# Attention and two feed-forward layers on one core: whole-tile query and key loads, sink values loaded head by head, and moved splits

## The reference

```python
# attention: q, k, v (2, 8, 768, 64); n_sink 4, window 128
scores = scale * np.matmul(q, k.transpose(0, 1, 3, 2))
keep = (pos[None, :] < n_sink) | ((rel >= 0) & (rel < window))
a = softmax(np.where(keep, scores, -1e9)); attn = np.matmul(a, v)
x = attn.transpose(0, 2, 1, 3).reshape(1536, 512)
# first layer: w_in (512, 1024), w_out (1024, 512)
h = x @ w_in
solu = h * softmax(h)
x = ((solu - mu) / np.sqrt(var + 1e-6) * g_ln) @ w_out
# second layer: w2_in (512, 2048), w2_out (2048, 512)
r = np.maximum(x @ w2_in, 0.0)
return (r * r) @ w2_out
```

## Time and profile before

| | us |
|---|---|
| median of 3 runs | 504.93 |
| lowest, highest | 503.52, 505.35 |
| the profiled execution's own time | 503.79 |
| its span | 502.1 |

### The profile page before, as it was taken

The page is one execution under the profiler, slowest core; times in us unless marked ns, Lnnn a source line. Parts: engine busy times, 40 slices in busy tenths (PEclk is TensorE's granted clock), DMA queues, the critical chain, the costliest instruction groups (busy, mean ns, idle before and its releaser), DMA issues.

```text
span 502.1 us, 7334 instructions
## 1 busy us (share of the span) xinstructions
PE 484.4 (96%) x2644; PEld 393.3 (78%) x2644; DVE 287.0 (57%) x513; ACT 201.1 (40%) x532; POOL 95.5 (19%) x138
## 2 busy tenths in 40 slices
PE   8989989999999999999789999999999999999997
PEld 6667667888778888877678888888888888888885
DVE  4999898888898887865693433332222232232222
ACT  3667546545665655433343322421211232221121
POOL 2555051120022202357970000000000000000000
PEclk9999999999999999999999999999999999999999
DMA  8921343452222211038100000020000002000002
GB/s 247 289 66 44 113 146 80 121 162 62 55 61 75 60 40 35 14 84 290 22 4 0 1 0 1 0 84 0 0 0 0 0 0 85 0 1 0 0 1 84
DMA packets 39717, 29.21 MB, mean 58 GB/s; under 512 B 29256, under 2 KB 29256, under 8 KB 39176
## 3 DMA queue, kind: packets, MB, share of 16 engines
q1 hardware_dynamic: 39384, 28.56, 19.6%
q10 hardware_dynamic: 304, 0.27, 0.2%
HBM read 22.52 MB, written 3.15 MB: 51 GB/s over the span
## 4 chain that ended last, share of the span: by engine, by line
PE 76%; DVE 14%; SPq 5%; ACT 2%; issue 2%; POOL 1%; DMA 0%; DVEq 0%; POOLq 0%; ACTq 0%
PE score_ps L1407 24%; PE h_ps L1419 12%; PE h_ps L1214 9%; PE w_ps L1252 7%; PE wt_ps L1419 6%; PE w_ps L1419 6%; SPq L342 4%; PE o_ps L1184 2%; PE score_ps L1156 2%; PE wt_ps L1164 1%; DVE prob L905 1%; PE wt_ps L1156 1%; DVE bstat L862 1%; SPq L399 1%; DVE u L855 1%
## 5 line engine op out<-in xcount | busy, mean ns | idle before, releaser
L1407 PE MATMUL score_ps<-x2T_hi,w2in_hi 128*128 (+1 forms) x192 | 74.8, 389 | 0.0
L1407 PE MATMUL score_ps<-x2T_hi,w2in_lo 128*128 (+1 forms) x192 | 74.7, 389 | 0.0
L1407 PE MATMUL score_ps<-x2T_lo,w2in_hi 128*128 (+1 forms) x192 | 74.7, 389 | 0.0
L1089 DVE TENSOR_TENSOR sq<-relu 128x512 f32<-128x512 f32 x24 | 18.6, 775 | 83.2 <-ACT relu L775 83.2
L1089 DVE TENSOR_TENSOR e<-e 128x512 f32<-128x512 f32 x24 | 18.5, 770 | 79.6 <-ACT e L775 79.6
L775 ACT ACTIVATE relu<-score_ps 128x512 f32<-128x512 f32 x24 | 14.4, 598 | 100.0 <-PE score_ps L1407 100.0
L775 ACT ACTIVATE e<-score_ps 128x512 f32<-128x512 f32 x24 | 14.4, 599 | 90.4 <-PE score_ps L1407 90.4
L1407 PEld LDWEIGHTS score_ps<-x2T_hi,w2in_lo 128*128 128x128 f32 x192 | 36.1, 188 | 7.5
L1407 PEld LDWEIGHTS score_ps<-x2T_hi,w2in_hi 128*128 128x128 f32 x192 | 36.0, 188 | 7.5
L1407 PEld LDWEIGHTS score_ps<-x2T_lo,w2in_hi 128*128 128x128 f32 x192 | 36.0, 188 | 7.3
L600 ACT ACTIVATE prob<-sm,nbias 128x132 f32<-128x132 f32 (+1 forms) x96 | 37.8, 396 | 0.5
(11 more groups left out here) (177 smaller groups left out, 1094.8 us busy)
## 6 DMA issues: line engine op xcount, KB each, us to landing
w2in<-w_in SPq DMA_DIRECT2D x4, 1024.0 KB, 5.1
w2out<-w_out SPq DMA_DIRECT2D x8, 512.0 KB, 7.4
V<-v SPq DMA_DIRECT2D x12, 256.0 KB, 2.7
x2T<-x SPq DMA_DIRECT2D x192, 16.0 KB, 1.8
k_raw<-kT SPq DMA_DIRECT2D x20, 132.0 KB, 2.8
q_raw<-qT SPq DMA_DIRECT2D x20, 128.0 KB, 2.8
w2in<-w_in SPq DMA_DIRECT2D x4, 512.0 KB, 6.5
w2in<-w_out SPq DMA_DIRECT2D x2, 1024.0 KB, 11.7
```

What stands on the lines that cost most here:

```text
L1089: nc.vector.tensor_tensor(sq[f % 2], relu[f % 2], relu[f % 2], ALU.mult).then_inc(sq_ready, 1)
L1407: done = mm(h2_ps[f % 2], ws[:, c, fs], xs[:, c, bass.ts(blk, BLK)], start=(c == 0 and i == 0), stop=(c == MC - 1 and i == 2))
```

## The change

It has five parts.

1. Queries and keys of a tile come with one DMA of 128 rows in place of two of 64: `by_halves` brings the halves of the heads to the front of the source pattern, whose dimensions are then 2 (halves), 64 (rows) and 512 or 528 values. Both early query tiles are issued by ScalarE.
2. `v_sink_raw` has 32 rows now. GpSimd clears it; then each head's four rows of 64 values come with a DMA of their own, 8 for a batch, 16 in all, issued after `w_out`. The mask `own_head` and its product are gone. GpSimd copies the rows twice and splits a third copy (`split_v_sink`), and does so for batch 0 ahead of `split_w_in(2)`.
3. ScalarE rounds queries and keys of tile 2 (before: GpSimd), and rounds chunk 3 of `w_in` earlier. VectorE normalises both groups of tile 1's probabilities ahead of splitting that chunk, and no longer splits `v_sink`.
4. In `second_step` some rows on TensorE and VectorE trade places.
5. At the start of stage B the last tile's squares go to `y[3]` in place of `x2`, so that they wait for no move, and stand ahead of `split_w2out(0)`; the later blocks' inputs are rounded and split at `f` = 7 and 11 in place of 2 and 4.

```diff
+X2T_AT = (7, 11)
...
+        def squares_of(t):
+            return y[3] if t == NT - 1 else x2[:, :]
...
-        def load_q01(queue, n, half):
-            rows, heads = half_heads(half)
-            queue.dma_start(q01[rows, n, :, :], qT[n, :, heads, :]).then_inc(q01_loaded[n], 16)
+        def by_halves(x):
+            return x.rearrange("d (a c) q -> a d c q", a=2)
+        def load_q01(queue, n):
+            queue.dma_start(q01[:, n, :, :], by_halves(qT[n])).then_inc(q01_loaded[n], 16)
...
-                for half in range(2):
-                    rows, heads = half_heads(half)
-                    sp.dma_start(q_raw[rows, :, :], qT[n, :, heads, :]).then_inc(q_loaded, 16)
+                sp.dma_start(q_raw[:, :, :], by_halves(qT[n])).then_inc(q_loaded, 16)
...
             def load_v_sink(b):
-                sp.dma_start(v_sink_raw[0:SKS, b, :],
-                             v[b * TPB, 0:N_SINK, :].unsqueeze(0).to_broadcast([SPLITS * H, N_SINK, DM])
-                             ).then_inc(v_sink_loaded[b], 16)
+                for place in range(H):
+                    rows, cols = slice(place * N_SINK, (place + 1) * N_SINK), slice(head(place) * D, (head(place) + 1) * D)
+                    sp.dma_start(v_sink_raw[rows, b, cols], v[b * TPB, 0:N_SINK, cols]).then_inc(v_sink_loaded[b], 16)
...
             load_w_out(1)
-            load_v_sink(1)
+            sp.wait_ge(sinks_cleared, 1)
+            for b in range(BATCH):
+                load_v_sink(b)
...
+            nc.gpsimd.memset(v_sink_raw[0:SK, :, :], 0.0).then_inc(sinks_cleared, 1)
+            def split_v_sink(b):
+                raw = v_sink_raw[0:SK, b, :]
+                pool.wait_ge(v_sink_loaded[b], 16 * H)
+                for part in range(2):
+                    nc.gpsimd.tensor_copy(v_sink[part * SK:(part + 1) * SK, b, :], raw).then_inc(v_sink_step, 1)
                 pool.wait_ge(v_sink_step, 2 * b + 2)
+                nc.gpsimd.tensor_tensor(v_sink[2 * SK:SKS, b, :], raw, v_sink[0:SK, b, :].bitcast(F32), ALU.subtract
+                                        ).then_inc(v_sink_ready, 1)
...
+            pool.wait_ge(w_split, 2)
+            split_v_sink(0)
             split_w_in(2)
-            build_v_sink(0)
-            round_v_sink(0)
-            round_k(2)
-            round_q(2)
...
-                if t:
+                if 0 < t < NT - 1:
                     dve.wait_ge(x2T_moved[(t - 1) // TB], (t - 1) % TB * MOVES + MOVES)
-                nc.vector.transpose(x2[:, :], x2_ps[:, :]).then_inc(x2_squared, 1)
+                nc.vector.transpose(squares_of(t), x2_ps[:, :]).then_inc(x2_squared, 1)
...
             chain(0, 0)
+            square_x2(NT - 1)
             split_w2out(0)
-            square_x2(NT - 1)
...
-                if f in (2, 4):
-                    split_x2T(f // 2)
+                if f in X2T_AT:
+                    split_x2T(X2T_AT.index(f) + 1)
```

More of the change, by code:

```diff
@@ L326, in load_k @@
                     sp.wait_ge(k_split, n - 1)
-                for half in range(2):
-                    rows, heads = half_heads(half)
-                    sp.dma_start(k_raw[rows, :, :], kT[n, :, heads, :]).then_inc(k_loaded, 16)
+                sp.dma_start(k_raw[:, :, :], by_halves(kT[n])).then_inc(k_loaded, 16)
             def load_v(n):
@@ L338, in move_x2 @@
                 sp.wait_ge(x2_squared, t + 1)
-                squares = x2[:, :].rearrange("p (c r b) -> p c r b", r=QUADS, b=SQ)
+                squares = squares_of(t).rearrange("p (c r b) -> p c r b", r=QUADS, b=SQ)
                 for i in range(QUADS):
@@ L353, in load_k01 @@
             def load_k01(n):
-                for half in range(2):
-                    rows, heads = half_heads(half)
-                    sp.dma_start(k01[rows, n, :, :], kT[n, :, heads, :]).then_inc(k01_loaded[n], 16)
+                sp.dma_start(k01[:, n, :, :], by_halves(kT[n])).then_inc(k01_loaded[n], 16)
             def load_v_sink(b):
-                sp.dma_start(v_sink_raw[0:SKS, b, :],
-                             v[b * TPB, 0:N_SINK, :].unsqueeze(0).to_broadcast([SPLITS * H, N_SINK, DM])
-                             ).then_inc(v_sink_loaded[b], 16)
+                for place in range(H):
+                    rows, cols = slice(place * N_SINK, (place + 1) * N_SINK), slice(head(place) * D, (head(place) + 1) * D)
+                    sp.dma_start(v_sink_raw[rows, b, cols], v[b * TPB, 0:N_SINK, cols]).then_inc(v_sink_loaded[b], 16)
             load_k01(0)
@@ L367, in _ @@
             load_k01(1)
-            for half in range(2):
-                load_q01(sp, 1, half)
             load_w_in(2)
-            load_v_sink(0)
             load_w_in(3)
@@ L412, in side_loads @@
         def side_loads(act):
-            for half in range(2):
-                load_q01(act, 0, half)
+            for n in range(2):
+                load_q01(act, n)
             act.dma_start(g_col[:, :], g_ln).then_inc(g_loaded, 16)
@@ L470, in _ @@
[L470 to L486, removed]
@@ L535, in _ @@
             halves(1, 1)
-            nc.gpsimd.tensor_tensor(QL[0][:, :, :], q_raw[:, :, :], QH[0][:, :, :].bitcast(F32), ALU.subtract
-                                    ).then_inc(q_split, 1)
             for t in range(NT - 1):
@@ L746, in _ @@
                 softmax_exp(1, h)
+            round_q(2)
+            round_k(2)
             copy_pT(1, 0)
@@ L1346, in second_step @@
                 project_0(True, 3, C1)
-                hidden(2, 16, 20)
                 score(3, 2)
                 score(3, 3)
+                hidden(2, 16, 20)
+                transpose_ln(1)
                 hidden(2, 20, 24)
-                transpose_ln(1)
                 project(1, 0, 16)
@@ L1383, in _ @@
             transpose_p(1, 0)
+            keep_warm(1)
+            transpose_p(1, 1)
             hidden_0(3, True)
             keep_warm(1)
-            transpose_p(1, 1)
-            keep_warm(2)
             first_step()
```

56 lines of the change are left out of this document (17 added, 39 removed).

## The result

The changed kernel takes 547.9 us (547.34 to 549.31, 4 runs) against 504.86 for the kernel before: ratio 1.0861, 95% interval 1.0831 to 1.0892. The forecast was 538.5, with a range of 514 to 558. The profiled execution has a span of 545.7 us and took 547.45.

The account below looks back on a forecast made before the run. TensorE, almost gapless from 72 us, and before that a softmax-TensorE chain were taken to bound it. 503.8 + 26.5 + 1.5 - 0.5 + 10 - 3.8 = 537.5; median 1.1 above the profiled execution: 538.5 us, range 514 to 558.

Parts of the forecast that it names:

- Two engines, the same ones: Query and key loads: outermost dimension 2 leaves each load two DMA engines, shared by all; 5.1 to 5.3 us per load.
- The rival with its own pair for each load: Two engines per load, but loads don't queue on each other: start +5.5, steps +10, 516 us; 7 in 100.
- those with 16 engines: Loads use 16 engines: sinks behind w_out, 505 to 507 us (6 in 100), or sinks early, 499 us (4 in 100).
- The start, +26.5 and +1.5 for the clock: To tile 1's last triangle: late loads and sinks +26.5 us; TensorE's clock falling back while idle +1.5, between 0 and 4.
- the landing of the sinks: Start: sink loads, behind w_out in the same queue, land at 46 us, and only then does GpSimd go on.
- the two engines' data end at 45.8: Start: summed work of early loads on the two engines, through tile 2's keys and queries, values and w_out, ends at 45.8.
- upper bound of +34: Start: +34 us if issuing holds up, 16 small sink issues at 0.6 us being 10 us.
- The start of tile 0's scores: Start: tile 0's keys and queries on two engines come by 13.4 us, so scores begin some 7.5 us later.
- The steady steps, +10: Seven query loads in the steps come later than needed, delaying xT_hi: about +10 us, bounds 5 and 15.
- Lands 7.6 us after issue: Steady steps: a query tile on two engines lands 7.6 us after issue; with 0.5 rounding, 8.1 us.
- Reordering, -0.5: Parts 3 and 4: gain only where VectorE's chain sets the pace, -0.5 us, between 0 and -1.
- Stage B, -3.8: Part 5: earlier last squares -2.3 us, later splits of block inputs -1.5; bounds of both -2.5 to -5.

Follow-up runs that it names:

- a_pairs: Changed kernel with every query and key load issued again as two DMAs of 64 rows, all else as changed: 506.07 us, ratio 1.0018.
- a_kpairs: Changed kernel with the key loads alone as two DMAs of 64 rows, queries still by halves: 541.57 us, ratio 1.0693.
- a_qpairs: Changed kernel with the query loads alone as two DMAs of 64 rows, keys still by halves: 520.53 us, ratio 1.0303.
- c_both: Changed kernel with query and key rows 128 outermost, sink loads ahead of w_out, and w_in's block 2 split ahead of batch 0's sinks: 501.11 us, ratio 0.9913.
- d_rows_B: Kernel before with single query and key loads of 128 rows outermost and the edits at stage B's start; sinks as before: 498.97 us, ratio 0.9865.
- a_one8: Changed kernel with query and key rows in memory in eight interleaved groups, so 8 outermost, still one DMA per load: 512.5 us, ratio 1.0136.
- a_one16: Changed kernel with query and key halves one behind the other in memory, so 128 rows outermost, still one DMA per load: 503.32 us, ratio 0.9955.
- a_sinks: Changed kernel, loads by halves kept, with the sixteen sink loads issued ahead of the third w_in block, not behind w_out: 541.64 us, ratio 1.0716.

## Why the prediction was right

**Two engines, the same ones.** Right, and shown: 2, 8 and 16 writes for outermost counts 2, 8 and 128, and 51 GB/s over both queues. The rival with its own pair for each load would have shown twice that; those with 16 engines came out in a_pairs (506.07, forecast 505 to 507).

**The start, +26.5 and +1.5 for the clock.** The mechanism was right and the sum 5.5 us short: tile 1's `xT_hi` begins 33.5 us later than before, where 28.0 were forecast. The term that was mis-sized is the landing of the sinks, 51.8 and not 46. The chain that ended last has nothing but SyncE's issues from 0.80 to 42.32, and goes on (start us, us, what; pieces between left out):

```profile
42.32 9.39 DMA v_sink_raw<-v
...
51.84 0.60 POOL v_sink L470
...
57.33 1.22 PE h_ps L1196 x2
```

TensorE has no part in it before 57.33, so no clock made the sinks late. GpSimd's part took 5.4 us (forecast 5.5). From there to the end of the last triangle are 6.4 us, 0.9 over the forecast's 5.5. With the two matmuls at 57.33 at 1.22 us for 0.62, that is most likely the clock's share of the path, inside its 0 to 4.

Why the sinks land late is shown in part. The forecast had the two engines' data end at 45.8. The rows are the rate in 40 slices of 3.0 to 47.6 us, and the sum of 48.6 to 50.4 us:

```profile
GB/s 290 337 300 234 52 50 54 52 52 49 52 54 51 96 314 197 298 155 49 50 49 49 52 51 52 49 49 79 238 236 358 272 272 332 281 169 60 51 52 51
```

```profile
DMA packets 82, 0.04 MB, mean 23 GB/s; under 512 B 66, under 2 KB 66, under 8 KB 82
```

The rate is never under 49 GB/s, that of two engines, up to 47.6, and falls away after about 48. Then come small packets, the sinks' rows and semaphore writes among them, until 50.2, and GpSimd starts at 51.84. As an estimate from these rows: some 2 us more for the data, 2.4 for the small packets and 1.6 until GpSimd starts, of which the forecast had none. My upper bound of +34 came near in size, but its reason was issuing that holds up the loads. SyncE did stand still (12.90, 4.48, 8.60, 3.29 and 8.42 us), yet no slice up to 47.6 shows the two engines short of work for it; in the stretches with wide loads the sum would hide that. The start of tile 0's scores, 16.39 and not 13.4, has the share of the wide loads on the two engines, which I had put behind the queries; this is the fit above.

**The clock in the steps is the other term, and I had put it at nothing.** I gave the clock +1.5 for the whole kernel, all in the start. TensorE's 4.7 us of extra busy time there lie mostly where it would have waited for loads anyway; about 0.9 is on the path. The steps have +3.0 (179.35 against 176.35 busy for the same 1231 matmuls, granted clock 0.97 in place of 1.00), with five waits for `lnT_lo` between them, 13.3 us in all and the longest 6.2. That such time adds to the steps is borne out by a_kpairs: about the same waits, 5.3 us more busy time, and steps that are 5.9 longer.

**The steady steps, +10.** They gave 14.3 where +9.5 was forecast: idle +11.3, with the reordering's -0.5 inside, and the clock's +3.0. a_qpairs and a_kpairs show that only the queries do it. "Lands 7.6 us after issue" was 7.3 to 9.3 from issue to rounding. Step by step, the seven that the forecast gave 4.2, 0, 2.8, 0.7, 1.1, 0 and 1.3 us took 5.9, 0.4, 1.8, 3.5, 1.0, 1.3 and 0 more than before. The sum is nearer than its terms, and that is partly luck.

**Reordering, -0.5.** a_pairs and a_qpairs measure -0.5 in the steps. In tile 1 it may cost once nothing else hides it (c_both).

**Stage B, -3.8.** It is -4.1 in eleven traces; TensorE's wait fell from 3.53 to 1.02, as forecast, to about 1.

**The 9.4 us by which the forecast was short.** They are 5.5 in the start and 4.8 in the steps, less 0.3 in stage B and less 0.6 because the median lies 0.45 above the profiled execution and not 1.1. Both large misses went the same way, so no error made good another.

**What stays open.** Why the steps cost 14.3 us in the changed kernel and 17.7 to 20.2 in the four others with query loads by halves: the waits are alike and the granted clock differs (0.97 against 0.95 or 0.96), but nothing here says why the same gaps lower it more. It is also open how much of the 2.9 us between c_both and d_rows_B is the sinks by heads and how much the order in tile 1, and what makes the two engines' data end some 2 us later than their bytes at 25.6 GB/s each.

## What to carry to other kernels

Before merging two DMAs into one, look at the outermost count of both patterns as the DMA will carry it, and lay the data out so that it is the 128 rows: the same merge cost 42 us with 2 outermost and gained 2.7 with 128. The count of packets of a queue tells how many engines a load uses, ahead of any timing. And where a loss makes TensorE idle for several us at a time, cost the matmuls behind each gap at the lower clock too, but only where TensorE is what is waited for: here that was 3.0 of 14.3 us in the steps, and 0.9 of 33.5 in the start, though TensorE's busy time grew by 4.7 there.

## What the runs showed of the hardware

- Loads on few engines hold up what is issued behind them: SyncE took 8.60 us for one issue of values and 12.90 for two of `w_in`, where 0.4 to 0.6 each is usual, and with eight engines still 7.06 us for two of `w_out`.
- The rate goes with the number of engines: 51 GB/s on two, 205 on eight (a_one8 from 22.8 to 26 us), and on sixteen 393 GB/s (a_one16 from 4 to 18 us, without a gap). The rows of eight and then of sixteen:

```profile
DMA packets 332, 0.66 MB, mean 205 GB/s; under 512 B 19, under 2 KB 19, under 8 KB 331
```

```profile
DMA  9999999999999999999999999999999999999999
...
DMA packets 2519, 5.50 MB, mean 393 GB/s; under 512 B 321, under 2 KB 321, under 8 KB 2519
```

- Sixteen small loads of 1 KB take SyncE 5.4 us (c_both) to 17.2 us (a_sinks) to issue. The loads are the same in both; what differs is what stands in the queue ahead of them.
